# Where the down products stand between the seven up products of a pair: twelve units regrouped in an fp32r feed-forward on one core

## The reference

```python
x = attention(q, k, v)                 # B=2, H=8, S=768, D=64; window and block sums
h = np.maximum(x.T @ w_tok1, 0) @ w_tok2
u = x + h.T                            # u: 2 batches x 768 rows x 512
y = u + np.maximum(u @ w_ch1, 0) @ w_ch2          # 512 -> 1536 -> 512
xn = layer_norm(y) * g_ln
out = y + np.maximum(xn @ w2_ch1, 0) @ w2_ch2     # 512 -> 2048 -> 512
```

## Time and profile before

| | |
|---|---|
| median of 3 runs | 580.57 us (579.64 to 581.44) |
| the profiled execution, its own time | 578.03 us |
| its span, first to last instruction | 576.2 us |
| PE busy | 563.0 us, 98% |
| PEld busy | 492.9 us, 86% |
| DVE busy | 351.0 us, 61% |
| POOL busy | 245.4 us, 43% |
| ACT busy | 225.1 us, 39% |
| granted TensorE clock, mean | 0.997 |
| PE's share of the chain that ended last | 89% |

### The profile page before, as it was taken

One profiled execution on the slowest core, in us unless ns is written; L12 is line 12 of the kernel. 1 busy time (PEld: TensorE's weight loads), 2 busy tenths in 40 slices (PEclk: granted clock), 3 DMA queues, 4 the chain that ended last, 5 costly groups with the idle time before them and its releaser, 6 DMA issues.

```text
span 576.2 us, 8223 instructions
## 1 busy us (share of the span) xinstructions
PE 563.0 (98%) x2905; PEld 492.9 (86%) x2905; DVE 351.0 (61%) x750; ACT 225.1 (39%) x418; POOL 245.4 (43%) x243
## 2 busy tenths in 40 slices
PE   8799999999999999999997999999999999999997
PEld 4678888889989888898986788898989898888986
DVE  6667556487667748548872674468865644444444
ACT  5688674663322252342244323633334212222220
POOL 4488663236554393080139963784459000000000
PEclk9999999999999999999998999999999999999999
DMA  8999620064555473344405184455374443333702
GB/s 257 271 233 249 192 91 2 19 255 165 201 202 201 168 274 129 150 157 165 148 19 195 41 277 163 169 196 178 151 292 164 165 164 123 137 128 144 237 1 109
DMA packets 21952, 94.81 MB, mean 165 GB/s; under 512 B 2344, under 2 KB 2472, under 8 KB 18328
## 3 DMA queue, kind: packets, MB, share of 16 engines
q1 hardware_dynamic: 21544, 93.62, 48.3%
q10 hardware_dynamic: 368, 0.67, 0.4%
HBM read 65.45 MB, written 28.84 MB: 164 GB/s over the span
## 4 chain that ended last, share of the span: by engine, by line
PE 89%; POOL 5%; DMA 2%; DVE 1%; issue 1%; ACT 0%; SPq 0%; ACTq 0%; POOLq 0%; DVEq 0%
PE bank L630 86%; POOL in_t L558 2%; DMA v_turned<-v_t 1%; DMA mask_sb<-mask 1%; PE bank L672 1%; PE bank L674 1%; PE bank L673 1%; DVE raw_in L1200 1%; PE bank L733 0%; POOL t_in L513 0%; POOL up_odd L499 0%; POOL up_even L499 0%; POOL t_in L511 0%; POOL up_odd L492 0%; POOL t_in L515 0%
## 5 line engine op out<-in xcount | busy, mean ns | idle before, releaser
L630 PE MATMUL bank<-down_w,hidden 128*128 128x512 f32 x1008 | 264.3, 394 | 0.0
L630 PEld LDWEIGHTS bank<-down_w,hidden 128*128 128x128 f32 x1008 | 186.7, 188 | 27.2
L968 ACT ACTIVATE hidden<-bank 128x384 fp32r<-128x384 f32 x112 | 55.1, 492 | 261.6 <-DVE bank L1165 191.9
L630 PE MATMUL bank<-in_t,up_even 128*128 128x384 f32 x588 | 119.5, 338 | 3.2 <-POOL in_t L558 3.2
L630 PE MATMUL bank<-in_t,up_odd 128*128 128x384 f32 x588 | 118.7, 336 | 0.8 <-DVE hidden L1157 0.5
L630 PEld LDWEIGHTS bank<-in_t,up_even 128*128 128x128 f32 x588 | 106.0, 189 | 12.4 <-issue 3.8
L630 PEld LDWEIGHTS bank<-in_t,up_odd 128*128 128x128 f32 x588 | 105.3, 188 | 10.4 <-POOL up_odd L492 0.9
L1157 DVE SCALAR_TENSOR_TENSOR hidden<-bank,hidden 128x384 fp32r<-128x384 f32 x112 | 62.4, 558 | 73.1 <-ACT hidden L968 72.8
L1165 DVE TENSOR_TENSOR bank<-bank,u 128x384 f32<-128x384 f32 x84 | 47.4, 565 | 19.9 <-PE bank L630 14.9
L1104 DVE CUSTOM_DVE_ANT_0 neg_scores<-bank,mask_sb 128x182 f32<-128x182 f32 x96 | 29.4, 344 | 26.7 <-PE bank L630 15.1
L1217 DVE TENSOR_TENSOR u<-bank,p 128x384 f32<-128x384 f32 x28 | 15.5, 555 | 44.3 <-PE bank L630 43.8
(11 more groups left out here) (100 smaller groups left out, 627.9 us busy)
## 6 DMA issues: line engine op xcount, KB each, us to landing
raw_down<-w_ch SPq DMA_DIRECT2D x28, 512.0 KB, 3.6
up_kept<-up_even SPq DMA_DIRECT2D x7, 1792.0 KB, 8.3
up_kept<-up_odd SPq DMA_DIRECT2D x7, 1792.0 KB, 8.2
up_even<-up_kept SPq DMA_DIRECT2D x7, 1792.0 KB, 7.3
up_odd<-up_kept SPq DMA_DIRECT2D x7, 1792.0 KB, 7.1
raw_up<-w_ch SPq DMA_DIRECT2D x14, 512.0 KB, 4.3
k_sb<-k_w SPq DMA_DIRECT2D x15, 273.0 KB, 6.6
v_own<-v_w SPq DMA_DIRECT2D x8, 390.0 KB, 4.2
```

The lines of the kernel that those rows point to most:

```text
L630: return nc.tensor.matmul(dst, lhs, rhs, start=start, stop=stop, skip_group_check=True)
L968: nc.scalar.activation(hidden[:, q % 2, f, 0, h * HN:(h + 1) * HN], src, ACT.Relu).then_inc(hid_high, 1)
```

## The change

The tuple of counts is replaced. The twelve units keep their order, each pair still runs all seven up products and twelve units, and every wait stays where it is; only the places of the units between the products move.

```diff
-DOWNS_AFTER = (1, 1, 2, 2, 2, 2, 2)
+DOWNS_AFTER = (0, 4, 0, 4, 0, 2, 2)
```

## The result

The changed kernel takes 588.66 us in the median of 4 runs (586.68 to 589.16), the kernel before 580.11 us beside it: a ratio of 1.0153, 95% interval 1.0126 to 1.018, or 8.6 us more. The forecast was 590.0 us (585.5 to 594.0), slower.

What follows compares the result with a forecast made beforehand. PE was taken to bound the kernel. Quarter 1's wait 7.9, full pairs 1.2, pair 6 0.8, start of group 2 1.5, less 1.9 given back, made +9.5 us: 590.0 us, range 585.5 to 594.0.

Steps and rivals of the forecast that it cites:

- The bound and the wait: PE sets a pair's time; product 6 newly waits for quarter 1's low part, made from product 4: 0.33 us a pair.
- The gain: Longer down runs and products 1 and 2 give back 0.08 us a pair, 1.9 us in 24 pairs.
- Full pairs: Pairs 9, 17 and 18, where DVE is busy without a break: u2 starts 0.39 us later, 1.2 us together.
- Pairs 6 and 7: Pair 6: 0.53 us more at product 6, and quarter 3 late for the next product 1, 0.28; together 0.8 us.
- Start of group 2: Pairs 10 to 12: POOL starts 0.8 us later, three down matmuls now come behind the wait, 0.7; together 1.5 us.
- rival one: The wait for quarter 1 is met after all, its chain from product 4 under 2.2 us: 578.5 us; chance 5%.
- rival two: Quarter 3 also misses product 1 of the next pair: 9.4 us more, 599.5 us; chance 7%.
- rival three: Small idle times lower PE's clock: 628 us if in each pair, 595 to 600 if in a few; chance 4%.

Runs made afterwards that it cites:

- a unit moved back: Against the changed kernel, one unit moved from behind product 3 to behind product 5: 582.47 us, ratio 1.0056.
- a shorter chain: The changed kernel's order with the sum behind product 4 (L1257) cut from 384 to 8 columns, for timing only: 580.42 us, one run.
- another order with as few runs: Counts (0, 2, 0, 4, 0, 4, 2) in place of the changed kernel's (0, 4, 0, 4, 0, 2, 2): 579.2 us, ratio 0.9991.
- the kernel with the late quarter 3: Against the changed kernel, one unit moved from behind product 6 to behind product 5: 589.95 us.
- the second twelve alone: Only the second half of the change against the kernel before, twelve down matmuls behind product 3 and none behind product 4: 585.0 us.
- one unit further: Against the changed kernel, one more unit moved from behind product 5 to behind product 3: 603.53 us.
- the added copy: One extra DVE copy of 384 columns between L1257 and the first add_c: 598.44 us in the changed order, 584.81 us in the order before.

## Why the prediction was right

**The bound and the wait.** Right, and now shown by taking it away from three sides: a unit moved back, a shorter chain, another order with as few runs. An ordinary pair was put at 15.69+0.33-0.08 = 15.94 and took 15.93.

**Its terms.** The wait was mis-sized by a little: 0.17 on the down matmuls and 0.12 on product 6, 0.29 for the 0.33. The first product behind a wait started 0.06 behind DVE's end, not 0.14, and then lost 0.12, not 0.08: with the 0.11 by which the chain is longer than the gap that makes the 0.29. (The 0.14 had been read in group 2. In the kernel with the late quarter 3, product 1 starts 0.06 behind DVE's end in groups 1 and 3 and 0.15 in groups 0 and 2, where it also waits on POOL; that the second wait makes the difference isn't shown.) The gain was too large by about as much, 0.08 for 0.05, and that the two cancelled in the pair's length is luck: runs of twelve gave their 0.04 a pair, but the 0.04 from up products did not come; it was read from products behind three down matmuls (1.06), and a pair of products behind twelve takes 2.11, just as slow. In the page's rule of a fixed cost per matmul ("TensorE: Matmul & The Clock Gate", section "Wait — 56ns, not 53.3ns?", the Trainium skill) nothing would be given back; the 15.64 of the kernel without a wait, for 15.69, says that a little is.

**Full pairs.** Put at 0.39 over the ordinary ones, they took 0.35 (16.28 to 16.29). The mechanism was the one named. What the prediction did not see is that it belongs to the first twelve alone; it was written as an addition to quarter 1's wait, and as such misled two of the later expectations.

**Pairs 6 and 7.** Together 0.61+0.55 over before, 0.7 over two ordinary losses, for the 0.8 said. In pair 7 product 1 starts 0.06 behind quarter 3's low part, the wait that was forecast there.

**Pair 2.** Missed. It lost 0.35 more than its neighbours. DVE's sum and `add_c` in it, changed kernel:
```profile
163.22 0.56 DVE L1257 TENSOR_TENSOR u<-bank,u 128x384 f32<-128x384 f32 x1 [0.86 <-PE bank L630]
164.25 0.57 DVE L1165 TENSOR_TENSOR bank<-bank,u 128x384 f32<-128x384 f32 x1 [0.47 <-PE bank L630]
```
The pause of 0.47, for 0.10 in all other pairs, stands at the same place in the kernel before (160.50 to 161.53), where the room in front of product 6 hid it. The runs bear that out: pair 2 loses the same 0.35 to 0.4 with the second twelve alone and with one unit further, and nothing extra in the orders that leave product 6 room. The pause stands in pair 2 of every profile without the added copy; what makes it wasn't found.

**Start of group 2.** Said 1.5 us for pairs 10 to 12 and 0.25 for pair 13, 1.75 in all; pairs 10 to 13 took 1.5 more together. POOL began 303.46-281.05 = 22.4 us into pair 10, for 21.7: 0.7 later, where 0.8 was said. It released product 1 of pair 13 32.9 us after that (336.35) as before (331.08, 33.0). From there to pair 14 it is 15.0 us for 14.1: the three down matmuls that now stand behind the wait, and pair 13's own wait for quarter 1. So POOL's path is as forecast. The sign named for it, product 1 of pair 13 about 1.1 us late, hardly shows in the first profile, where PE itself came late out of pair 12, at a low clock for longer; in the second profile it does. The weight loads of that product, first and second profile:
```profile
336.35 0.99 PEld L630 LDWEIGHTS bank<-in_t,up_odd 128*128 128x128 f32 x6 [0.17 <-POOL up_odd L499]
```
```profile
336.34 0.99 PEld L630 LDWEIGHTS bank<-in_t,up_odd 128*128 128x128 f32 x6 [1.16 <-POOL up_odd L499]
```
The date is the same to 0.01 us, whenever PE arrives.

**Rivals.** In no pair was the wait for quarter 1 met ahead of time (rival one). Its price of 578.5 was wrong besides: the kernel with the short chain is that case, and it took 580.42 us in its one run, 1.4 us over the kernel before from pair 1 to pair 27, since the price left the full pairs and the start of group 2 out. Product 1 was on time in ordinary pairs, 0.46 to 0.48 us behind quarter 3's low part and in pairs 6 and 20 0.22 (rival two, but see the kernel one unit away), and the clock did not fall at the small waits (rival three): from pair 1 to pair 11, with a wait in every pair, the stretch has a granted clock of 1.00, and so has the one from 351.3 to 559.0 us, pairs 14 to 26 (PE, PEld, DVE, ACT, POOL busy; clock; DMA).
```profile
136.32:297.33 161.01, 159.44 (x781) 140.20 (x780) 106.34 (x187) 51.30 (x84) 63.98 (x52) 1.00 0.50 177
```
The Trainium skill's warning of micro-idles ("TensorE: Matmul & The Clock Gate", section "A second HAM failure mode: psum-queue depth-cycling") is not borne out at some 0.4 us of idle weight loads per 16 us, nor at the 0.70 us of PE per 16.6 of the kernel with one unit further (granted clock 1.00 from 339 to 573 us of its span); the measurement decides.

**Sum.** +9.5 said, +8.6 by the medians, +9.2 by the profiles without the attention part. Part of the closeness is misses that cancel: pair 2's 0.35, not foreseen, against 0.2 to 0.3 too much for the ordinary pairs, 0.2 at the start of group 2 and 0.2 in the full pairs and pairs 6 and 7.

## What to carry to other kernels

When filler work is moved on the bounding engine, list for each wait what stands between the work that starts its chain and the wait, in microseconds, and compare with the chain's length: the loss is the difference, one for one, plus a small price for the release (0.18 us here), and the count of runs or switches hardly matters. Moving filler ahead of a producer also makes everything behind that producer late in the helper engine's queue, which shows only in the stretches where that queue is full. A stable pause on a helper engine, hidden today, comes out as soon as the cover is spent.

## What was not expected of the hardware

**The same idle, three lengths of low clock.** At the start of pair 12 PE is idle for some 3.1 us in the three profiles below, and what follows differs; no pattern was found. The changed kernel's two profiles, then the one of the order before with the added copy (PE's timelines):
```profile
316.44 4.18 PE L630 MATMUL bank<-in_t,up_even 128*128 128x384 f32 x12 [3.02 <-POOL in_t L558]
320.42 3.95 PE L630 MATMUL bank<-down_w,hidden 128*128 128x512 f32 x12
324.20 2.27 PE L630 MATMUL bank<-in_t,up_even 128*128 128x384 f32 x12
```
```profile
316.39 4.07 PE L630 MATMUL bank<-in_t,up_even 128*128 128x384 f32 x12 [3.04 <-POOL in_t L558]
320.30 2.90 PE L630 MATMUL bank<-down_w,hidden 128*128 128x512 f32 x12
323.04 2.27 PE L630 MATMUL bank<-in_t,up_even 128*128 128x384 f32 x12
```
```profile
315.14 1.28 PE L630 MATMUL bank<-in_t,up_even 128*128 128x384 f32 x6 [3.17 <-POOL in_t L558]
316.26 0.86 PE L630 MATMUL bank<-down_w,hidden 128*128 128x512 f32 x3
```
At full speed twelve up matmuls take 2.09 us and twelve down matmuls 2.76. In the first profile they took 3.98 and 3.78 (granted clock 0.50 from 316.44 to 322.30), in the second of the same program 3.91 (with a short wait of product 1 in it) and 2.74, and in the third kernel six up matmuls took 1.12, at full speed after an idle time no shorter. Over the study the low clock (1.2 GHz) cost between nothing and 2.9 us there. In the changed kernel's two profiles none of the difference reached the total: POOL releases product 1 of pair 13 at 336.35 either way, so a longer stretch of low clock only shortens PE's wait for it.

**DVE's copy behind POOL.** A copy of 384 float32 columns between SBUF tiles took 0.35 us alone and 0.67 to 2.36 us where it began under POOL's L499; in all 19 such cases of the two kernels it ended 0.21 or 0.22 us after L499, wherever it had begun, while `add_c`, with one operand in PSUM, kept its 0.55 to 0.57 wherever it stood beside the same instruction. DVE's low part of the down weights, with two operands in SBUF, took 1.21 us alone and up to 2.90 beside POOL (pair 19 of the changed kernel). The Trainium skill's "GPSIMD Engine Reference", section "1. Specifications", says that SBUF interfaces are shared with VectorE, with contention for DVE's two-port modes or two SBUF inputs; the trace agrees in that the copy and the down weights' low part were longer beside POOL and `add_c` was not; whether the copy runs in a two-port mode isn't shown. Its ends show that it isn't slowed but held until POOL is through.
